# Banded attention, a skip-gated mixture and an expert-choice mixture: setup and attention written as one unrolled pipeline

## The reference

```python
# attention: B, H, S, D = 4, 8, 768, 64; n_global = 8, n_local = 96
scores = q @ k.T / sqrt(D)
keep = (key < n_global) | ((0 <= row - key) & (row - key < n_local))
scores += -slope[h] * dist          # |row - key|; n_local for a global key outside the band
a = exp(scores - max) over kept keys;  a /= sum(a) + 1e-9
x = a @ v                           # regrouped to x[3072, 512]
# mixture 1: rows with x @ w_skip > 0 go to the expert argmax(x @ w_gate), 8 experts
out = x + gate * (relu(x @ w1[e]) @ w2[e])
# mixture 2: each expert takes its 384 best rows (greedy over sorted logits)
y[rows of e] = relu(x @ w1[e]) @ w2[e]
```

## Time and profile before

| what | us |
|---|---|
| median of 3 runs (lowest to highest) | 983.8 (982.5 to 985.3) |
| the profiled execution | 987.73 |
| its span, first to last instruction | 986.0 |
| TensorE busy in the span | 794.3 |
| VectorE, ScalarE, GpSimd busy | 551.8, 490.6, 192.9 |
| mean granted TensorE clock | 0.930 |

### The profile page before, as it was taken

The page is one execution under the profiler, slowest core; times in us unless marked ns, Lnnn a source line. Parts: engine busy times, 40 slices in busy tenths (PEclk is TensorE's granted clock), DMA queues, the critical chain, the costliest instruction groups (busy, mean ns, idle before and its releaser), DMA issues. The chain is left out here.

```text
span 986.0 us, 18432 instructions
## 1 busy us (share of the span) xinstructions
PE 794.3 (81%) x5547; PEld 710.0 (72%) x5547; DVE 551.8 (56%) x1414; ACT 490.6 (50%) x1103; POOL 192.9 (20%) x259
## 2 busy tenths in 40 slices
PE   0478888877884469999999991269999899999995
PEld 0477877877884469889898981158878788788794
DVE  4467475574762456656666640667466575664420
ACT  0588686886972045545445530053535535354450
POOL 1100010010010022222222213023131432313321
PEclk9999999999988569999999995579999999999998
DMA  3998889799714435555554301156766567677850
GB/s 56 214 189 187 235 193 224 184 185 282 156 44 135 170 119 198 192 198 204 195 188 170 130 14 21 71 168 183 189 235 171 172 182 203 219 186 246 205 107 36
DMA packets 111532, 164.02 MB, mean 166 GB/s; under 512 B 36454, under 2 KB 64358, under 8 KB 111472
## 3 DMA queue, kind: packets, MB, share of 16 engines
q1 hardware_dynamic: 93232, 114.96, 41.4%
q0 software_dynamic: 11968, 35.74, 15.1%
q10 hardware_dynamic: 6272, 12.58, 3.4%
HBM read 125.86 MB, written 23.76 MB: 152 GB/s over the span
## 5 line engine op out<-in xcount | busy, mean ns | idle before, releaser
L931 ACT ACTIVATE pr<-pr,nmx 128x232 f32<-128x232 f32 (+1 forms) x192 | 88.7, 464 | 12.9 <-DVE nmx L1006 11.5
L1484 PE MATMUL r_ph<-r_xh,r_w1h 128*128 128x384 f32 x256 | 90.5, 353 | 0.0
L844 PE MATMUL tp<-ident,pr 128*128 128x128 f32 x352 | 59.5, 289 | 38.0 <-ACT pr L931 38.0
L832 PE MATMUL sc<-kk,qh 128*128 128x256 f32 x192 | 59.7, 332 | 36.3 <-DVE ql L993 36.3
L1484 PE MATMUL r_ph<-r_xh,r_w1l 128*128 128x384 f32 x256 | 86.3, 337 | 0.0
L1484 PE MATMUL r_ph<-r_xl,r_w1h 128*128 128x384 f32 x256 | 86.0, 336 | 0.0
L360 PE MATMUL m_ph<-m_xh,m_w1h 128*128 128x256 f32 x288 | 84.2, 292 | 0.9 <-issue 0.9
L360 PE MATMUL m_ph<-m_xl,m_w1h 128*128 128x256 f32 x288 | 81.9, 284 | 0.0
L360 PE MATMUL m_ph<-m_xh,m_w1l 128*128 128x256 f32 x288 | 81.8, 284 | 0.0
L420 ACT ACTIVATE m_hh<-m_ph 128x256 fp32r<-128x256 f32 x72 | 27.7, 384 | 108.1 <-PE m_ph L360 98.8
L991 DVE TENSOR_TENSOR kk<-k_raw,kk 64x1288 fp32r<-64x1288 f32 x32 | 48.1, 1503 | 55.6 <-ACT kk L919 55.2
(11 more groups left out here) (246 smaller groups left out, 2124.4 us busy)
## 6 DMA issues: line engine op xcount, KB each, us to landing
m_w<-moe_w SPq DMA_DIRECT2D x18, 2048.0 KB, 8.4
r_w<-moe_w SPq DMA_DIRECT2D x32, 512.0 KB, 6.1
r_w<-moe_w SPq DMA_DIRECT2D x8, 2048.0 KB, 9.6
r_w2l<-r_w POOLq DMA_DIRECT2D x32, 512.0 KB, 5.1
q_raw<-qT SPq DMA_DIRECT2D x32, 384.0 KB, 5.8
x_rows<-xb ACTq DMA_DIRECT2D x8, 1536.0 KB, 8.9
k_raw<-kT SPq DMA_DIRECT2D x64, 160.0 KB, 4.4
k_raw<-kT SPq DMA_DIRECT2D x64, 120.0 KB, 4.5
```

Source lines behind the costliest of these rows:

```text
L832: nc.tensor.matmul(to, qh[s][:, hh, q], kk[s][:, hh, keys], start=True, stop=False)
L844: last = nc.tensor.transpose(tp[m % 2][:, c * P:(c + 1) * P], parts[c], ident[:])
L931: nc.scalar.activation(pr[n % 4][:, t, lo:CW], pr[n % 4][:, t, lo:CW], ACT.Exp, bias=nmx[n % 4][:, t:t + 1], scale=-1.0, accum_out=sums[hd ...
L1484: last = nc.tensor.matmul(ph[m % 4][:, 0:CAP], w[:, c, m * P:(m + 1) * P], x[:, c, :], start=(c == 0 and a == 0), stop=(c == KC - 1 and a ...
```

## The change

- Setup and attention become one block. SP issues the two limits first, then the first pairs' loads, then the tables. VectorE builds masks as soon as the limits and the first nine GpSimd fills are there; the biases of head `h+1` are made in step `h`. ScalarE runs one exponential (`spark`) at the start.
- The loop over batches is gone: 96 units, 106 steps in all, are written out for each engine.
- The host lays keys out as `kI`: each tile's 128 keys, with the eight global keys behind it (`KW` = 832), so that 232 columns in a row hold the band. Two transfers a pair load it. Global value rows come as `vG`. GpSimd has no work in the loop.
- Behind the values stand 64 columns of ones. A value product takes 64 value columns and those 64, so the row sum stands in column 64 of each tile's 72-column place (`OW`); `exps` has no `accum_out`.
- `pr` has six buffers for four, `prt` four for three; transposes run 3 steps behind scores for 2.
- The gate is cut into 32 pieces, two for each pair, with three transposes, one copy of 384 columns and three products of 64 columns. They share the transpose banks and `prt` with the units, in one numbered order (`unit_item`, `gate_item`), and add up in `lp` over a batch's four pairs.
- `xb` has two buffers, stored from SP, and stays allocated to the end of mixture 1; the wait for the stores moves to the router's SP.

```diff
+KW = QT_N * (P + FAST_GLOBAL) + 16
+OW = D + 8
...
-        attention = ExitStack()
...
-            @block.sync
-            def _(sp):
-                sp.dma_start(ints[:, 0:1], n_global.partition_broadcast(P)).then_inc(loaded, 16)
...
-                sp.wait_ge(loaded, 7 * 16)
...
+        late = ExitStack()
+        xb = [late.enter_context(nc.sbuf_tensor(f"xb{s}", [P, QT_N, DM], F32)) for s in range(2)]
+        stored = late.enter_context(nc.semaphore("x_stored"))
...
-            pr = [tb(f"pr{s}", [P, 2, CW]) for s in range(4)]
-            prt = [tb(f"prt{s}", [P, 512]) for s in range(3)]
...
+            V_OWN, V_BAND = 2 * QT_N, 2 * (QT_N - 1)
+            vo = [tb(f"vo{s}", [P, (V_OWN + 1) * D]) for s in range(2)]
+            vp = [tb(f"vp{s}", [CA, (V_BAND + 1) * D]) for s in range(2)]
+            PRS, PRTS, LAG = 6, 4, 3
+            pr = [tb(f"pr{s}", [P, 2, CW]) for s in range(PRS)]
+            prt = [tb(f"prt{s}", [P, 512]) for s in range(PRTS)]
+            nmx = [tb(f"nmx{s}", [P, 2]) for s in range(PRS)]
...
+            PAIRS, PARTS, RAW_LOADS, V_LOADS, TABLE_LOADS = B * H // 2, 4, 4, 3, 5
+            ALL_UNITS, HEADS = B * UNITS, B * H
+            STEPS = ALL_UNITS + LAG + 7
+            RELS, FILLS = 9, 25
+            def norm_step(hd):
+                return 3 * hd + LAG + 4
+            def gate_step(q):
+                return norm_step(2 * (q // 2) + 1) + 2 + q % 2
+            unit_item, gate_item = {}, {}
+            for n in range(STEPS):
+                if 0 <= n - LAG < ALL_UNITS:
+                    unit_item[n - LAG] = len(unit_item) + len(gate_item)
+                for q in range(2 * PAIRS):
+                    if gate_step(q) == n:
+                        gate_item[q] = len(unit_item) + len(gate_item)
+            def turned_in(n):
+                units = [n - LAG] if 0 <= n - LAG < ALL_UNITS else []
+                return units, [q for q in range(2 * PAIRS) if gate_step(q) == n]
...
-                return vo[s][:, (QT_N * hh + i) * D:(QT_N * hh + i + 2) * D]
+                x = QT_N * hh + i
+                return vo[s][:].rearrange("p (x d) -> p x d", d=D)[:, x:V_OWN + 1:V_OWN - x, :]
...
+                def load_raw(g):
+                    s = g % 2
+                    if g >= 2:
+                        sp.wait_ge(part_low[s], PARTS * (g // 2))
+                    for half in range(2):
+                        w = slice(half * D, half * D + D)
+                        sp.dma_start(k_raw[s][w], kI[g].rearrange("h d n -> d h n")).then_inc(raw_loaded[s], 16)
+                        sp.dma_start(q_raw[s][w], qT[g].rearrange("(h d) n -> d h n", h=2)).then_inc(raw_loaded[s], 16)
+                def load_v(g):
+                    s = g % 2
+                    if g >= 2:
+                        sp.wait_ge(used, unit_item[6 * (g - 2) + 5] + 1)
+                    bands = vp[s][:, 0:V_BAND * D]
+                    sp.dma_start(vo[s][:, 0:V_OWN * D], vL[g]).then_inc(v_loaded[s], 16)
+                    sp.dma_start(bands[0:FAST_LOCAL, :].rearrange("p (h m) -> p h m", h=2),
+                                 vL[g, P - FAST_LOCAL:P].rearrange("p (h m) -> p h m", h=2)[:, :, 0:(QT_N - 1) * D]).then_inc(v_loaded[s], 16)
+                    sp.dma_start(bands[FAST_LOCAL:CA, :], vG[g]).then_inc(v_loaded[s], 16)
+                def store(b):
+                    sp.wait_ge(normed, H * (b + 1))
+                    for dst in (x_dram, x1_dram):
+                        sp.dma_start(dst[S * b:S * (b + 1), :].rearrange("(i p) d -> p i d", p=P), xb[b % 2][:]).then_inc(stored, 16)
...
+                load_raw(0)
+                load_v(0)
+                load_raw(1)
+                sp.dma_start(wg1_cols[:, :, 0:E + 1], w_gate1.rearrange("(c p) e -> p c e", p=P)).then_inc(loaded, 16)
+                sp.dma_start(wg1_cols[:, :, E + 1:], w_gate2.rearrange("(c p) e -> p c e", p=P)).then_inc(loaded, 16)
+                load_v(1)
...
+                    for g in range(2, PAIRS):
+                        load_raw(g)
+                        if g >= 3:
+                            load_v(g - 1)
+                        if g >= 6 and g % 4 == 2:
+                            store(g // 4 - 1)
+                    load_v(PAIRS - 1)
+                    store(B - 1)
...
-                    with sp.Fori(0, B) as b:
-                        for j in range(H // 2):
-                            s, use = j % 2, 2 * b + j // 2
-                            q2, k2, v2 = pair((H // 2) * b + j)
-                            at(sp, part_low[s], PARTS * use)
-                            for half in range(2):
-                                w = slice(half * D, half * D + D)
-                                k_own, k_src = k_raw[s][w], k2.rearrange("(h d) n -> d h n", h=2)
-                                sp.dma_start(k_own[:, :, 0:P], k_src[:, :, 0:P]).then_inc(raw_loaded[s], 16)
...
+                        at_key = (P + FAST_GLOBAL) * i - CA if i else 0
+                        keys = slice(at_key, at_key + 256)
...
+                def turn_gate(q):
+                    item, g = gate_item[q], q // 2
+                    pe.wait_ge(normed, 2 * g + 2)
+                    if item >= 2:
+                        pe.wait_ge(kept, item - 1)
+                    rows, c = xb[g // 4 % 2], g % 4
+                    for t in range(3):
+                        last = nc.tensor.transpose(tp[item % 2][:, t * P:(t + 1) * P], rows[:, 3 * (q % 2) + t, c * P:(c + 1) * P], ident[:])
+                    last.then_inc(turned, 1)
...
+                        o = op[hd % 2][:, i * OW:i * OW + 2 * D].rearrange("p (x d) -> p x d", d=D)
...
+                def gate_products(q):
+                    item, g = gate_item[q], q // 2
+                    b, c = g // 4, g % 4
+                    pe.wait_ge(kept, item + 1)
+                    if q == 0:
+                        pe.wait_ge(loaded, 2 * 16)
+                    if c == 0 and b and q % 2 == 0:
+                        pe.wait_ge(read, b)
+                    for t in range(3):
+                        i = 3 * (q % 2) + t
+                        last = nc.tensor.matmul(lp[:, i * D:(i + 1) * D], prt[item % PRTS][:, t * P:(t + 1) * P],
+                                                wg1[:, c * G1:c * G1 + D], start=(c == 0 and i == 0), stop=(c == KC - 1 and i == QT_N - 1))
+                    last.then_inc(used, 1)
...
+                    pe.wait_ge(filled, FILLS)
+                    for n in range(STEPS):
+                        if n < ALL_UNITS:
+                            scores(n)
+                        units, gates = turned_in(n)
+                        for m in units:
+                            turn_unit(m)
+                        for q in gates:
+                            turn_gate(q)
+                        units, gates = turned_in(n - 1)
+                        for m in units:
+                            values(m)
+                        for q in gates:
+                            gate_products(q)
...
-                                             accum_out=sums[hd % 4][:, 2 * u + t:2 * u + t + 1]).then_inc(exped, 1)
...
+                def keep(item, w):
+                    act.wait_ge(turned, item + 1)
+                    if item >= PRTS:
+                        act.wait_ge(used, item - PRTS + 1)
+                    nc.scalar.activation(prt[item % PRTS][:, 0:w], tp[item % 2][:, 0:w], ACT.Copy).then_inc(kept, 1)
...
+                    for n in range(STEPS):
+                        if n < ALL_UNITS:
+                            exps(n)
+                        units, gates = turned_in(n + 1)
+                        for m in units:
+                            keep(unit_item[m], 3 * P if m % 3 == 0 else 4 * P)
+                        for q in gates:
+                            keep(gate_item[q], 3 * P)
+                        g, c = n // 6 + 1, n % 6 - 1
+                        if g < PAIRS and 0 <= c < PARTS:
+                            split(g, c)
...
+                def norm(nlink, hd):
+                    b = hd // H
+                    parts = op[hd % 2][:, 0:QT_N * OW].rearrange("p (i c) -> p i c", c=OW)
+                    dve.wait_ge(used, unit_item[3 * hd + 2] + 1)
+                    nlink(v.tensor_scalar(sums[hd % 2][:], parts[:, :, D], 1e-9, None, ALU.add))
+                    nlink(v.reciprocal(rcp[hd % 2][:], sums[hd % 2][:]))
+                    if hd % H == 0 and b >= 2:
+                        dve.wait_ge(stored, 32 * (b - 1))
+                    h = hd % H
+                    v.tensor_tensor(xb[b % 2][:, :, h * D:(h + 1) * D], parts[:, :, 0:D],
+                                    rcp[hd % 2][:].unsqueeze(2).broadcast_to([P, QT_N, D]), ALU.mult).then_inc(normed, 1)
...
+                def take_logits(b):
+                    dve.wait_ge(used, gate_item[2 * (4 * b + 3) + 1] + 1)
+                    v.tensor_copy(logits[:, QT_N * b:QT_N * (b + 1), :],
```

(58 more changed lines are left out.)

405 lines of the change are left out of this document (149 added, 256 removed).

## The result

The changed kernel takes 922.3 us (median of four, 916.9 to 923.5) against 984.6 (982.5 to 989.0): ratio 0.935, 95% interval 0.930 to 0.940, so 62.3 us less where 81.2 were forecast. The forecast of 903 was 19 us too low; the range of 889 to 925 holds the time. The profiled execution took 922.9 us with a span of 921.0.

A forecast was written before the change was run, and what follows sets the result against it. The bound was to pass from ScalarE (12.2 us per pair) to TensorE (12.3, gate inside): 13.9 start, 196.2 work, 4.0 clock, 2.0 and 2.8 ramps, 7.9 stalls make 226.8 against 308.0, 81.2 less; on the median 903 us, range 889 to 925.

The forecast's parts named there:

- the likeliest case: Whole kernel: TensorE bound as summed, 903 us, own range 895 to 911; chance 0.52.
- rival (c): Attention: three engines hold each other up, stalls 10 to 14% instead of 4, 915 to 923 us; chance 0.22.
- rival (d): Attention loads: store queue's rate not reached, 14.5 us per pair holds, 35 us less gained, 930 to 940; chance 0.07.
- the sum: Start to last logits copy: terms total 226.8 us against 308.0, so the profiled execution falls from 987.7 to 906.5.
- I take the first, since packets grow fourfold: Attention transfers: 3.1 MB a pair at 390 GB/s, 8 us inside 12.3, rather than 14.5 at 211 GB/s.
- if they land at 12.5 the start is 15: Start: fallback if the first pair's loads land at 12.5 us, not near 10; first scores 15, not 13.9.
- half-clock start: Start of attention: first matmuls at the 1.2 GHz level for at least 8 us, costing 4.0 us.
- ramps: Attention's ends: ramp-in 2.0 us before the first maxima, ramp-out 2.8 us behind the last values.
- 4% of stalls: Attention on TensorE: stalls of 4% of its 196.2 us of work, 7.9 us.
- Nothing: End of attention: last store lands while the router works, and SP's new wait for it costs nothing.
- rival (e): Unrolled attention: instruction fetch stalls eat the gain from 5 us per pair on; at twice that 1065 us; chance 0.03.
- From the logits copy on, the same length: Sign for everything behind the last logits copy: unchanged at 678 us.

The follow-up runs named there:

- the control: k0_control: the changed kernel unedited, run again on a second chip; 918.8 us, ratio 0.932 to the kernel before.
- e3: Against the changed kernel: a pair's two heads side by side in longer key and query rows, still transfers into 64 partitions; 917.6 us, ratio 0.932 to before.
- e2: Against the changed kernel: key and query arrays doubled by the host, one transfer each into all 128 partitions; 922.1 us, ratio 0.937 to before.
- e1: Against the changed kernel: the last batch's two stores issued by the router's SP, behind its logits store; 917.0 us, ratio 0.933 to before.
- e4: Against the changed kernel: four probability buffers, three transposed ones, transposes two steps behind scores; 917.8 us, ratio 0.933 to before.
- e5: Against the changed kernel: the exponentials' accumulator reads of row sums put back; 921.0 us, ratio 0.935 to before.
- e10: e2 with the edits of e1 and e4; 916.2 us, ratio 0.930 to the kernel before.
- e11: e10 with the doubled key and query arrays declared behind the expert weights, same instructions; 906.9 us, ratio 0.917 to the kernel before.
- e9: e3's 64-partition transfers, reading half of e2's doubled input arrays; 930.6 us, ratio 0.945 to the kernel before.

## Why the prediction held, and what was off

The time lies in the range and outside the likeliest case's own 895 to 911. It falls among the 915 to 923 of rival (c), but the mechanism is a weak form of rival (d), whose times the range leaves out. That the range holds the time is in part luck: it had been widened for other causes. The profiled execution was 922.9 - 906.5 = 16.4 us above the sum:

- **Loads: +11.4 (8.8 by the control).** This is the step that failed: "I take the first, since packets grow fourfold". The changed kernel's packets had grown, and the rate stayed: 232 GB/s with stores. Neither end was right for a whole pair. From the first batch's copy to the third's (88.5 to 195.4 us, eight pairs) a pair takes 13.4 us, and at a share of 0.97 that is 13.0 us of the transfer engines, where 8 were summed and 14.5 stood as the other end. Keys and queries (1.64 MB into 64 partitions) are 7.6 of it at e3's 216 GB/s; stores and values (0.79 + 0.64 MB) are the other 5.4, not the 3.7 that 390 GB/s would give. With 128 partitions, e2, a pair takes (185.3 - 84.0) / 8 = 12.7 us by the same two copies, and 0.64 of that is 8.1 us, the number in the sum. The earlier trace rows held the answer: there the slow queue wrote halves of the tile and the fast one read whole tiles, and I put the difference down to packet size. The trace of before, sorted by packet size (60 to 290 us), says so without a run: the load queue's packets of 3072 bytes took 212 ns, 232 GB/s over 16 engines, and those of 512 bytes 39 ns, 212 GB/s. e2 against e3 shows the cause. The price of rival (d), 35 us, was too high: it had 14.5 us of transfers a pair for 13.0, and so 2.2 us a pair lost where 13.4 - 12.7 = 0.7 were.
- **The start: +2.8.** The limits land 1.2 later than forecast, the first pair's queries at 13.5 and not near 10; the case "if they land at 12.5 the start is 15" was nearer.
- **TensorE's work and stalls: -4.** e2 starts 2.6 late and ends the stage 1.2 early, so work, half-clock start, ramps and 4% of stalls were 3.8 us too much together. A gate pass is 0.10, not 0.11.
- **The last store: +3.1.** "Nothing" was wrong: it lengthens the step from the stage to the router (e1), from 3.3 us before to 6.4. What in that step waits for it is not shown.
- **The rest behind the copy: +2.9.** Mixture 2 takes 4.8 us more (306.5 to 311.3) and the rest 1.9 less; executions of one kernel differ by as much (4.3).

These add to 11.4 + 2.8 - 4.0 + 3.1 + 2.9 = 16.2; the time around the span is 0.2 longer.

Point by point: the bound moved to TensorE, but two pairs take 26.7 us where about 25 were forecast; with wide loads (e2) they take 25.3, the 12.3 plus 4% a pair of the sum. Batch ends leave no gap: right. ScalarE's key split waits for loads, 7.5 us in five waits: the prediction called that a sign of being wrong, and what it points at, the loads, is the step that failed. Waits for exponentials under 10: right in number, and the reason given, distance and buffers, wrong (e4): depth was not needed. ScalarE off the bound: right; the reads alone were worth about 2.3 us (e5). Of the 71.0 us up to the copy, 36.3 - 16.7 = 19.6 are the earlier first scores. Most of the other 51.4 must be from the gate and the batch ends inside the pipeline, which no run separates. Instruction fetch, rival (e): no idle time of such a kind shows (TensorE's waits above have no row without a releaser). "From the logits copy on, the same length": off by 6.0.

**Rival (c)** is not needed: in e10 and e11 TensorE is busy 99% (60 to 210 us) with the shallow buffers, so three engines at these loads do not hold each other up by 10%.

The changed kernel can be bettered: e11_arrays_last, 906.9 us, by wide key and query loads, a later last store, a smaller distance and depth, and the large arrays declared last.

## What to carry to other kernels

When two queues of a profile run at different rates, compare everything in which they differ, partitions touched and direction too, before crediting packet size; an experiment that changes one of them costs one run. Read off the transfer share after an unrolling: engines that stop waiting for each other soon wait for loads. And read the stages that were not edited: a gain of 11 us in one stage was given back whole in another, when larger inputs were declared ahead of its weights (e2).

## What had not been expected of the hardware

- **The place of an array in memory is worth 1%.** In the three kernels that declare doubled keys and queries ahead of the weights, m_w's 2 MB land in 9.5 to 9.6 us and mixture 2 takes 319 to 322 us; in all ten other variants they land in 8.4 to 8.6, and it takes 307 to 313. e9 puts the loss in without a change of the transfers, e11 takes it out with the same bytes. Which property of the address does it stays open; no run moved one array by a chosen amount.
- **Late weights cost more than the wait.** In e9 against e3 mixture 2 takes 10.5 us more. TensorE's wait for `r_fullf` grows by 5.4 us, ScalarE's for the second weights (`r_w2h`) by 6.3; that the first comes of the second is not shown. The same 2078 matmuls also take longer: from 578 us to behind the last of them (908 in e3, 918 in e9) TensorE is busy 314.5 us against 310.3 and idle 25.5 against 19.7. The granted clock over 580 to 700 us is 0.94 against 0.97, so the 4.1 us of longer work is likely clock.
- **A repeated source as the outermost dimension** ran at 52 GB/s in two engines' time, and made the kernel 372 us longer than its control.
